# Weight remainders on one engine, small activation remainders on another, in a fused attention and two-MLP kernel

## The reference

```python
f = 1.0 / (1.0 + np.exp(-f_logit))
for t in range(S):                       # gated linear attention, a state of 48 x 48 per head
    state = f[:, :, t, :, None] * state + np.einsum('bhd,bhe->bhde', k[:, :, t], v[:, :, t])
    y[:, :, t] = np.einsum('bhd,bhde->bhe', q[:, :, t], state)
x = y as (3072, 384)
x = (sigmoid(x @ w_gate) * (x @ w_val)) @ w_out      # first MLP
h = x @ w_in;  out = (h * sigmoid(1.702 * h)) @ w_out2   # second MLP
```

## Time and profile before

| | us |
|---|---|
| runs shown | 967.09 (median), 965.51, 1323.11 |
| the profiled execution | 964.99 |
| its span | 963.3 |
| TensorE busy | 934.1 (97%) |
| VectorE busy | 493.7 (51%) |
| ScalarE busy | 349.5 (36%) |
| GpSimd busy | 152.4 (16%) |
| longest waits of TensorE, in total: first hidden product for ScalarE's sigmoid | 12.1 in 7 |
| the same for GpSimd's k_dec, and for VectorE's scores | 2.8 in 3, 2.3 in 1 |

### The profile page before, as it was taken

One profiled execution on the slowest core, in us unless ns is written; L12 is line 12 of the kernel. 1 busy time (PEld: TensorE's weight loads), 2 busy tenths in 40 slices (PEclk: granted clock), 3 DMA queues, 4 the chain that ended last, 5 costly groups with the idle time before them and its releaser, 6 DMA issues.

```text
span 963.3 us, 18025 instructions
## 1 busy us (share of the span) xinstructions
PE 934.1 (97%) x7219; PEld 781.0 (81%) x7219; DVE 493.7 (51%) x872; ACT 349.5 (36%) x797; POOL 152.4 (16%) x174
## 2 busy tenths in 40 slices
PE   7888998999999999999999999999999999999997
PEld 5777897888888888888888888888888888888885
DVE  8976867655655765565333234343343443443433
ACT  3454453343434433333324333333332233233332
POOL 4443332221221221112004430000000000000000
PEclk9989999999999999999999999999999999999999
DMA  6642232211221211121032330020010100100000
GB/s 162 181 141 67 74 81 70 59 44 43 75 62 51 67 52 52 44 71 30 21 107 68 97 115 1 1 66 0 1 66 1 54 13 1 65 1 1 33 1 35
DMA packets 44007, 52.35 MB, mean 54 GB/s; under 512 B 8464, under 2 KB 33808, under 8 KB 43920
## 3 DMA queue, kind: packets, MB, share of 16 engines
q1 hardware_dynamic: 41184, 43.30, 15.5%
q10 hardware_dynamic: 2736, 7.85, 2.8%
HBM read 36.96 MB, written 9.44 MB: 48 GB/s over the span
## 4 chain that ended last, share of the span: by engine, by line
PE 85%; DVE 6%; issue 3%; ACT 2%; SPq 2%; DMA 1%; POOL 0%; ACTq 0%; DVEq 0%; POOLq 0%
PE up_ps L1052 16%; PE up_ps L1054 16%; PE up_ps L1053 16%; PE out_ps L1052 12%; PE out_ps L1053 11%; PE out_ps L1054 11%; PE att_ps L1003 1%; DVE prod L782 1%; SPq L402 1%; DVE act_lo L900 1%; DVE w_lo L842 1%; PE att_ps L1025 1%; PE att_ps L1045 1%; DVE inv_prod L789 1%; PE att_ps L1015 1%
## 5 line engine op out<-in xcount | busy, mean ns | idle before, releaser
L1052 PE MATMUL up_ps<-x_hi,w_hi 128*128 128x512 f32 (+1 forms) x792 | 295.1, 373 | 13.3 <-ACT act_f L695 12.1
L1054 PE MATMUL up_ps<-x_hi,w_lo 128*128 128x512 f32 (+1 forms) x792 | 294.5, 372 | 0.0
L1053 PE MATMUL up_ps<-x_lo,w_hi 128*128 128x512 f32 (+1 forms) x792 | 294.4, 372 | 0.0
L1052 PE MATMUL out_ps<-act_hi,w_hi 128*128 128x512 f32 (+1 forms) x540 | 208.6, 386 | 1.1 <-DVE act_lo L900 1.1
L1053 PE MATMUL out_ps<-act_lo,w_hi 128*128 128x512 f32 (+1 forms) x540 | 203.5, 377 | 0.0
L1054 PE MATMUL out_ps<-act_hi,w_lo 128*128 128x512 f32 (+1 forms) x540 | 203.1, 376 | 0.0
L701 ACT CAST act_hi<-act_f 128x512 fp32r<-128x512 f32 (+1 forms) x180 | 106.6, 592 | 249.6 <-DVE act_f L891 177.1
L900 DVE TENSOR_TENSOR act_lo<-act_f,act_hi 128x512 fp32r<-128x512 f32 (+1 forms) x180 | 126.1, 700 | 116.0 <-ACT act_hi L701 116.0
L1052 PEld LDWEIGHTS up_ps<-x_hi,w_hi 128*128 128x128 f32 x792 | 150.6, 190 | 40.1 <-issue 10.9
L1054 PEld LDWEIGHTS up_ps<-x_hi,w_lo 128*128 128x128 f32 x792 | 150.8, 190 | 25.4
L1053 PEld LDWEIGHTS up_ps<-x_lo,w_hi 128*128 128x128 f32 x792 | 150.8, 190 | 25.1
(11 more groups left out here) (77 smaller groups left out, 581.0 us busy)
## 6 DMA issues: line engine op xcount, KB each, us to landing
stage<-w SPq DMA_DIRECT2D x16, 384.0 KB, 3.3
stage<-w ACTq DMA_DIRECT2D x9, 576.0 KB, 4.3
q_raw<-q_t SPq DMA_DIRECT2D x96, 48.0 KB, 1.9
k_raw<-k_t SPq DMA_DIRECT2D x96, 48.0 KB, 1.9
v_raw<-v_n SPq DMA_DIRECT2D x48, 96.0 KB, 2.2
x_raw<-x_dram SPq DMA_DIRECT2D x6, 768.0 KB, 4.7
out_t<-final SPq DMA_DIRECT2D x18, 256.0 KB, 2.3
f_raw<-f_t SPq DMA_DIRECT2D x82, 48.0 KB, 1.9
```

Of the source, the lines that this page charges most:

```text
L1052: pe.matmul(dst, w_hi[:, at:at + P], m_hi, start=first, stop=False)
L1053: pe.matmul(dst, w_hi[:, at:at + P], m_lo, start=False, stop=False)
L1054: return pe.matmul(dst, w_lo[:, at:at + P], m_hi, start=False, stop=last)
```

## The change

VectorE makes the remainders of all weight pieces but piece 0: `by_pool` and `split_w1_piece` go, and block j's call of `w1_second_part(j + 2)` stands in all of blocks 0 to 9. GpSimd makes the activation remainders of the 24 small blocks (`split_act`, SMALL) instead of VectorE, with a semaphore of their own. The scores' part of y is no longer copied by ScalarE and added by GpSimd: VectorE adds it from PSUM (`add_y(n, v)`, behind the new states), and a later visit waits for that addition instead of ScalarE's copy. In group 0 the gates and decays are made in other blocks: the decay of unit 7 in block 3 instead of 1, and so on to unit 11 in block 11 instead of 9. ScalarE takes y after the gates and the weight cast in group 0. Ahead of the blocks some calls change places on ScalarE, VectorE, GpSimd and SyncE. In groups 0 to 5 x's third slab is cast and its remainder made in block 11 instead of 10; there on VectorE it stands behind `prepare`. Left out below: the lines that declare or drop semaphores and the tile y_scores.

```diff
@@ -46 +46 @@
     BLOCKS1 = NG1 * J1
+    SMALL = 2 * J1
@@ -71 +72 @@
         if g == 0:
-            forgets = {j: n + 2 for n, j in enumerate((0, 1, 2, 4, 6, 8))}
-            prepares = {j: n + 1 for n, j in enumerate((0, 1, 3, 5, 7, 9))}
+            forgets = {j: n + 2 for n, j in enumerate((0, 1, 4, 6, 8, 10))}
+            prepares = {j: n + 1 for n, j in enumerate((0, 3, 5, 7, 9, 11))}
         else:
...
@@ -262 +262 @@
-        def by_pool(t):
-
-            return t > 1 and t % 2
-
         def wait_w1(eng, t):
@@ -270 +266 @@
                 eng.wait_ge(w1_thirds, 3)
-            elif by_pool(t):
-                eng.wait_ge(w1_pool_split, len([s for s in range(t + 1) if by_pool(s)]))
             else:
-                eng.wait_ge(w1_split, len([s for s in range(1, t + 1) if not by_pool(s)]))
+                eng.wait_ge(w1_split, t)
+
+        def wait_act_split(eng, q):
+
+            if q < SMALL:
+                eng.wait_ge(first_act_split, q + 1)
+            else:
+                eng.wait_ge(act_split, q - SMALL + 1)
@@ -286 +287 @@
             if out_visit[n] < BEFORE_MLP:
-                eng.wait_ge(y_taken, n + 1)
+                eng.wait_ge(y_copied, n + 1)
             else:
@@ -440 +441 @@
                 load_kq(6)
-                load_kq(7)
                 load_f(8)
+                load_kq(7)
@@ -500 +501 @@
-                def decay(n):
-                    if n >= UNITS:
-                        return
+                def decay_q(n):
                     u = Unit(n)
@@ -509 +508 @@
                     pool.tensor_tensor(q_dec[:, n % 4, :], q_raw[:, u.s, :], prod[:, u.s, :], ALU.mult).then_inc(q_dec_done, 1)
+
+                def decay_k(n):
+                    u = Unit(n)
                     pool.wait_ge(k_loaded[u.s], (u.uses + 1) * 32)
@@ -515 +517 @@
+                def decay(n):
+                    if n < UNITS:
+                        decay_q(n)
+                        decay_k(n)
+
                 def split_w1(part):
@@ -523 +530 @@
-                def split_w1_piece(t):
+                def split_act(b):
-                    piece = slice(t * PIECE1, (t + 1) * PIECE1)
-                    pool.wait_ge(w1_hi_done, t + 1)
-                    pool.tensor_tensor(w_lo[:, piece], w1_staged(t), w_hi[:, piece].bitcast(F32),
-                                       ALU.subtract).then_inc(w1_pool_split, 1)
-
-                def add_y(n):
-                    pool.wait_ge(y_taken, n + 1)
-                    pool.tensor_tensor(y_t[:, n % YS, :], y_t[:, n % YS, :], y_scores[:, n % 2, :], ALU.add).then_inc(y_added, 1)
+                    pool.wait_ge(act_hi_done, b.q + 1)
+                    pool.tensor_tensor(act_lo[:, b.t, 0:b.n], act_f[:, b.t, 0:b.n], act_hi[:, b.t, 0:b.n].bitcast(F32),
+                                       ALU.subtract).then_inc(first_act_split, 1)
@@ -550 +552 @@
                 split_w1(1)
-                decay(4)
+                decay_q(4)
+                pool.wait_ge(state_done, states_before(4))
                 split_w1(2)
+                decay_k(4)
                 decay(5)
@@ -556 +560 @@
                     for j in range(J1):
-                        if g == 0 and j + 2 < J1 and by_pool(j + 2):
-                            split_w1_piece(j + 2)
-                        if (g, j) in VISIT_AT and VISITS[VISIT_AT[g, j]][2] is not None:
-                            add_y(VISITS[VISIT_AT[g, j]][2])
+                        if g * J1 + j < SMALL:
+                            split_act(BLOCK[g * J1 + j])
                         if (g, j) in PREPARE_AT:
@@ -622 +624 @@
                     wait(act, y_moved[n % YS], 16 * moves(n % YS, n))
-                    scores_part = banks(v)[:, :, Y_COL:STATE_COL].rearrange("p r (c t) -> p c r t", c=BLOCKS)
                     y = y_t[:, n % YS, :].rearrange("p (c r t) -> p c r t", c=BLOCKS, r=SIDES)
                     if v < BEFORE_MLP:
-                        act.copy(y, scores_part).then_inc(y_taken, 1)
+                        act.copy(y, banks(v)[:, :, Y_COL:STATE_COL].rearrange("p r (c t) -> p c r t", c=BLOCKS)).then_inc(y_copied, 1)
                         return
@@ -629 +630 @@
                         for r in range(SIDES):
-                            act.copy(y[rows[i], :, r, :], banks(v)[rows[r], i, STATE_COL:STATE_COL + BLOCKS * C].rearrange(
+                            last = act.copy(y[rows[i], :, r, :], banks(v)[rows[r], i, STATE_COL:STATE_COL + BLOCKS * C].rearrange(
                                 "p (c t) -> p c t", c=BLOCKS))
-                    wait(act, y_added, n - 1 - UG)
-                    act.copy(y_scores[:, n % 2, :].rearrange("p (c r t) -> p c r t", c=BLOCKS, r=SIDES),
-                             scores_part).then_inc(y_taken, 1)
+                    last.then_inc(y_copied, 1)
-                def x_first_part(group):
+                def x_first_part(group, slabs=range(KC)):
                     wait(act, act_used, hidden_blocks_before(group - 1))
@@ -640 +639 @@
                         act.wait_ge(x2_loaded, 16 * (group - NG1 + 1))
-                    for k in range(KC):
+                    for k in slabs:
                         if group < NG1:
@@ -677 +676 @@
                 first_move_y(2, slice(2, None))
-                w1_first_part(1)
                 take_y(3)
                 first_move_y(3, slice(0, 1))
-                w1_first_part(2)
+                w1_first_part(1)
                 load_w1(3)
@@ -684 +682 @@
                 x_first_part(0)
+                w1_first_part(2)
                 load_w1(4)
@@ -692 +691 @@
                         act.wait_ge(hid_ready, q - BLOCKS1 + 1)
-                    wait(act, act_split, q - 1)
+                    if q >= 2:
+                        wait_act_split(act, q - 2)
                     if b.first_mlp:
@@ -701 +701 @@
                     act.copy(act_hi[:, b.t, 0:b.n], act_f[:, b.t, 0:b.n]).then_inc(act_hi_done, 1)
+                    turned = made = None
                     if b.first_mlp and (b.g, b.j) in VISIT_AT:
                         turned, _, made = VISITS[VISIT_AT[b.g, b.j]]
-                        if turned is not None:
-                            take_k(turned)
-                        if made is not None:
-                            take_y(made)
+                    if turned is not None:
+                        take_k(turned)
+                    if made is not None and b.g:
+                        take_y(made)
                     if b.first_mlp and (b.g, b.j) in FORGET_AT:
@@ -714 +715 @@
                             load_w1(b.j + 5)
+                        if made is not None:
+                            take_y(made)
                     if b.first_mlp and b.g < NG1 - 1 and b.j == SPLIT_AT1:
-                        x_first_part(b.group + 1)
+                        x_first_part(b.group + 1, range(KC - 1))
+                    if b.first_mlp and b.g < NG1 - 1 and b.j == SPLIT_AT1 + 1:
+                        x_first_part(b.group + 1, [KC - 1])
                     if b.group >= NG1 - 1 and b.group < NG1 + NB - 1 and b.j == SPLIT_AT2:
@@ -822 +827 @@
+                def add_y(n, v):
+
+
+                    dve.wait_ge(y_copied, n + 1)
+                    y = y_t[:, n % YS, :].rearrange("p (c r t) -> p r c t", c=BLOCKS, r=SIDES)
+                    dve.tensor_tensor(y, y, banks(v)[:, :, Y_COL:STATE_COL].rearrange("p r (c t) -> p r c t", c=BLOCKS),
+                                      ALU.add).then_inc(y_added, 1)
+
                 def after_visit(v):
@@ -829 +842 @@
                         new_states(kept, v)
+                    if made is not None and v >= BEFORE_MLP:
+                        add_y(made, v)
@@ -880 +895 @@
                 end_decay(4)
-                w1_second_part(1)
-                after_visit(7)
                 begin_decay(5)
+                w1_second_part(1)
                 x_second_part(0)
+                after_visit(7)
                 end_decay(5)
@@ -895 +910 @@
                                           ALU.mult).then_inc(mul_done, 1)
-                    if b.q < J1 and b.j + 2 < J1 and not by_pool(b.j + 2):
+                    if b.q < J1 and b.j + 2 < J1:
                         w1_second_part(b.j + 2)
+                    if b.q >= SMALL:
-                    dve.wait_ge(act_hi_done, q + 1)
-                    dve.tensor_tensor(act_lo[:, b.t, 0:b.n], act_f[:, b.t, 0:b.n], act_hi[:, b.t, 0:b.n].bitcast(F32),
-                                      ALU.subtract).then_inc(act_split, 1)
+                        dve.wait_ge(act_hi_done, q + 1)
+                        dve.tensor_tensor(act_lo[:, b.t, 0:b.n], act_f[:, b.t, 0:b.n], act_hi[:, b.t, 0:b.n].bitcast(F32),
+                                          ALU.subtract).then_inc(act_split, 1)
                     v = VISIT_AT.get((b.g, b.j)) if b.first_mlp else None
@@ -909 +925 @@
                     if b.first_mlp and b.g < NG1 - 1 and b.j == SPLIT_AT1:
```

(19 more changed lines are left out.)

## The result

The changed kernel takes 969.1 us (median of 22 runs, 965.67 to 975.39), the one before on the same chip 965.75 (22 runs, the 1323.11 of the table above among them): a ratio of 1.004, 95% interval 1.0025 to 1.0054. Within 2% it is no change, as forecast; but it is slower and not faster, and 5.3 us above the 963.8 predicted: 1.2 us gained were forecast, 3.4 were lost between the medians. The profiled execution is one of 972.36 us (span 970.6), 7.4 above the one of before and 3.3 above its own kernel's median.

What follows compares the result with a forecast made beforehand. TensorE was taken as full from 149.4 to 950.5 us, leaving about 16 us idle in groups 0 and 1 plus half clock. +2.4 + 5.8 - 2.0 + 4.7 - 2.5 - 6.2 - 1.0 = 1.2 gained: 964.99 to 963.8, range 955.5 to 969.

Steps and rivals of the forecast that it cites:

- Half clock: Group 0: slow products after each visit now lie on the path; charged 1.0 us loss, bounds 0 and 3.
- Start: Ahead of block 0: costed at nothing, bounds -0.5 and +0.5 us, since the same y transfers end it.
- Blocks 0 to 3: Group 0's first blocks: 19.0 us becomes 13.2, gain 5.8, as a decay and a GpSimd weight piece leave.
- Pairs: Group 0, blocks 3 to 9, three pairs of blocks: 10.7 us a pair against 11.5, gain 2.4.
- Group 1: Blocks 12 to 23: 53.9 us becomes 49.2, gain 4.7, VectorE dropping act_lo and ScalarE y_scores.
- Start of group 2: After block 23: x's last slab behind that block's decay, a 2.0 us pause at slab 2; loss 2.5.
- Boundaries: Groups 2 to 4 into the next: last slab behind block 11's decay pauses TensorE 2.06 us each; loss 6.2.
- GpSimd's hold before the scan: Group 0: GpSimd's act_lo gets in between VectorE's weight split and scan; charged 0.46 us each time.
- A: Rival, slower: boundary pauses stay 6.2 us, slow-clock chain makes group 0's pairs 11.5 again; 968 us, chance 0.2.
- B: Rival, front gains more: no GpSimd hold, half clock free, group 1 nearer TensorE's pace; 958.5 us, chance 0.2.
- C: Rival: no pause at the boundaries, slab and decay being in time; 957.6 us, chance 0.05.
- D: Rival: nothing measurable moves, VectorE in group 0 trading GpSimd's 2.65 us for 1.45 of its own; 965 us, chance 0.1.

Runs made afterwards that it cites:

- after_again: The changed kernel itself, unaltered, run again beside all_fillers on the same chip: 971.41 us, ratio 1.0058 to the kernel before.
- all_fillers: Changed kernel with 7 to 9 useless products in each TensorE pause of about 2 us (visits of blocks 4, 6, 8; slab 2 of groups 1 to 5): 961.9 us.
- filler: Changed kernel with 12 useless products in TensorE's pause ahead of slab 2 at groups 3 to 5: 968.89 us, ratio 1.003 to the kernel before.
- slab_back: Changed kernel with all three x slabs made in block 10 again, on ScalarE and VectorE: 955.68 us, ratio 0.9886 to the kernel before.
- act_vector: spread_old with all activation remainders on VectorE again: 955.57 us, ratio 0.9897 to the kernel before.
- w_gpsimd: spread_old with the odd weight pieces' remainders on GpSimd again: 953.22 us, ratio 0.9872 to the kernel before.
- y_gpsimd: spread_old with y's scores copied by ScalarE and added by GpSimd again: 953.09 us, ratio 0.9873 to the kernel before.
- slab_only: The kernel before with only x's last slab moved a block later: 976.27 us, ratio 1.0103 to the kernel before.
- decay_first: slab_back with the decay ahead of the weight split on VectorE in blocks 3, 5, 7 and 9: 951.65 us, ratio 0.9843 to the kernel before.
- slab_first: Changed kernel, last slab still in block 11 but ahead of gates on ScalarE and decay on VectorE: 957.11 us, ratio 0.9903 to the kernel before.
- filler8: filler with 8 instead of 12 useless products in each pause: 968.79 us, ratio 1.002 to the kernel before.
- visit_filler: slab_back with nine useless products ahead of the visits of blocks 4, 6 and 8: 953.76 us, ratio 0.9869 to the kernel before.
- spread_old: slab_back with group 0's gates and decays in the blocks of the kernel before: 951.18 us, ratio 0.984 to the kernel before.

## Why the prediction was wrong

**The step that failed is "Half clock ... I charge 1.0 (bounds 0 and 3)".** It measured 9.5 between the medians of after_again and all_fillers (7.2 against the first 969.1), outside the bounds either way. Without it the sum of the other terms is 1.2 + 1.0 = 2.2 us gained, 962.8; the kernel without it takes 961.9. That they agree so well is in part luck: the start, 1.5 late in that profile, and the boundaries, 0.6 over, are made up by four terms that came out 0.3 to 0.8 better; and from the before of its own session (965.47) it is 3.6 gained, of which the profiles have 1.2 behind multiplication 60, where nothing was forecast. In the profiles half clock is 5.9 us in the three pairs (37.6 against 31.7) and 4.7 at the three boundaries (267.0 against 262.3). Two faults made it so small. The first is the size in group 0. The prediction itself said that slow products had been "partly free" and "are on the path" now, and yet took 1.0 of bounds up to 3. In the kernel before they were wholly free: its three pairs last 11.5 us each, the first two with half clock in them and the third without.

```profile
50.72:62.24 11.52, 9.68 (x120) 9.10 (x120) 8.69 (x15) 5.57 (x14) 4.87 (x5) 0.85 0.50 145
62.24:73.73 11.49, 9.67 (x120) 9.25 (x120) 8.67 (x15) 5.67 (x14) 4.84 (x5) 0.85 0.52 150
73.73:85.24 11.51, 8.43 (x120) 7.81 (x120) 8.69 (x14) 5.57 (x14) 4.87 (x5) 1.00 0.23 68
```

After, they are the chain: one stretch of 17 products at 0.21 instead of 0.12 is 1.5 us, and the profile has 13.6 us of half clock in the three pairs, some four such stretches. The second fault is that the term was put on group 0 alone: new pauses of 2 us in stages that had had none and a clock of 1.00 were priced at their own length, although in group 0 of the kernel before half clock comes right behind a pause of 1.83 us (at 62.3; not behind one of 1.82, at 73.8).

**The other terms.** Start: costed at nothing (bounds 0.5), measured 1.2 late; slabs 1 and 2 of x waited for y's transfers (0.71 and 0.58 us on ScalarE). It differs between executions, from 31.7 to 33.6 over the profiles, and in filler, whose code is the changed kernel's up to there, it is 31.74; so it is not put down to the change. Blocks 0 to 3: gain 5.8 said, 6.0. Pairs: 10.7 said, 10.56 without half clock. Blocks 9 to 12: loss 2.0, 1.2. Group 1: gain 4.7, 5.0. Start of group 2: loss 2.5, 2.4. Boundaries: 2.06 each said; with fillers 2.14 each, 6.4 for three (84.52 to 86.66 for the first), and half clock adds 1.5 to 1.7 to each. The 6.8 from 24 to 60 has 0.35 more, which slab_back, without these pauses, has too (255.86 against 255.51).

**Where the engines share.** GpSimd's hold before the scan was charged 0.46; it is 0.55 in blocks 3, 5, 7 and 9 (1.23 against 0.68). The Trainium skill ("SBUF — State Buffer", who interferes with whom) has the engine that issues first keep the pair for its whole instruction; the order agrees with the rows (GpSimd starts in VectorE's split and gets through between split and scan), the price lies between the 0.46 charged and the 0.73 that its rule would give, and for the five of group 0 neither is off by more than 1 us.

**The rivals.** A, the slower one at 968, came nearest in time: its 11.5 a pair was 12.1 to 13.5. But it let half clock lengthen only the visits' chain, and left the boundaries at 6.2 where they cost 11.5. B is refuted by the scan rows and by all_fillers (half clock is not free), C by the pauses, D by the slab's move (13.4 us) and the small remainders (act_vector, 4.4), which move time and in part cancel; for w_gpsimd and y_gpsimd that is not shown.

**Where the gain went.** The change did what it says: the sigmoid no longer waits and the front is 2.9 us ahead at block 24 (150.97 against 153.91), in spite of half clock. Then three boundaries take back 3.6, 3.8 and 4.1.

## What to carry to other kernels

A new pause of TensorE is not priced by its length: look in the trace at what products cost behind pauses of the same size, and charge that for each, wherever it falls, above all in stages that were full: here a pause of 1.83 us cost 3.6 to 4.1 in the profile. Work for the next stage goes ahead of work that is not due yet on an in-order queue; a slab a block later was harmless (957.1 against 955.7, not told apart), the same slab behind a decay costs 1%. When parts of a change pull in both directions, a kernel for each part shows what to keep: here the change without two of its parts is 1.6% faster than the kernel before.

## What the runs showed of the hardware

- Pauses of 1.83 us on TensorE, in a stream at 2.4 GHz, were each followed, 0.3 to 1.5 us behind their end, by 3.4 us at 1.2 GHz in the profiles of the changed kernel, of after_again and of slab_only (nine pauses). The Trainium skill ("TensorE: Matmul & The Clock Gate", HAM oscillation) tells of such an oscillation from bursts with longer waits between them; the shorter pauses are what the rows add. Not every pause is followed by it: 1.60 in decay_first and 1.14 in slab_first were not, nor was the one of 2.34 to 2.37 at the start of group 2 in the changed kernel, after_again, filler and filler8, and of slab_back's three pauses of 2.4 the first was not (10.58 for that pair). What decides between them was not settled.
- Products whose result nobody reads, in the place of the pause, keep the clock at 1.00 behind it (filler, filler8, visit_filler, all_fillers). A 128x128 float32 one is two records and takes 0.24 us; eight cost nothing in the pause at a boundary (the next product starts 2.22 after the last real one, with them and without), twelve overran.
- GpSimd's 256-column remainder is 0.74 us alone and 1.35 to 1.82 where it meets VectorE's (changed kernel); VectorE's four state products are 1.64 instead of 1.18 where it comes upon them (spread_old, block 6).
